# Last products with V moved ahead of router work at the end of attention, and three low pieces of the first weights moved behind the first index lists

## The reference

```python
# attention, 8 heads of 64: keys within 16 positions, and 24 blocks of 32 keys (max of k, mean of v)
a = softmax(concat(mask(scale * q @ k.T), scale * q @ k_sum.T + log(32)))
x = a @ concat(v, v_sum)
# first mixture: 8 experts, the best two of noisy logits
logits = x @ w_gate + log1p(exp(x @ w_noise)) * noise
for e in range(8):                      # top2_w: softmax over the two
    out[mask] += top2_w * (relu(x[mask] @ w1[e]) @ w2[e])
# second mixture: one expert per token, and only where x @ w_skip > 0; out = x + gate * expert(x)
```

## Time and profile before

| | |
|---|---|
| median of 3 runs | 667.83 us (665.47 to 668.64) |
| the profiled execution's own time | 665.87 us |
| its span in the profile | 663.4 us |
| PE busy | 620.8 us, 94% of the span |
| DVE busy | 367.9 us, 55% |
| ACT busy | 293.9 us, 44% |
| POOL busy | 237.9 us, 36% |

### The profile page before, as it was taken

One profiled execution on the slowest core, in us unless ns is written; L12 is line 12 of the kernel. 1 busy time (PEld: TensorE's weight loads), 2 busy tenths in 40 slices (PEclk: granted clock), 3 DMA queues, 4 the chain that ended last, 5 costly groups with the idle time before them and its releaser, 6 DMA issues.

```text
span 663.4 us, 13555 instructions
## 1 busy us (share of the span) xinstructions
PE 620.8 (94%) x4054; PEld 551.5 (83%) x4054; DVE 367.9 (55%) x714; ACT 293.9 (44%) x536; POOL 237.9 (36%) x223
## 2 busy tenths in 40 slices
PE   6888848999999999999999999998699999999994
PEld 6567735999999999999999999985478888888883
DVE  5759985644535554364644536423564687656641
ACT  2657732433424443253433434433255475646621
POOL 2558303105527063370725527033112223231230
PEclk9999967999999999999999999998699999999998
DMA  9999881442926448283672926885296679568220
GB/s 305 326 285 305 301 295 53 155 152 55 269 66 180 140 93 264 54 213 94 150 207 54 273 65 157 236 251 113 72 330 208 208 220 357 160 187 266 40 50 13
DMA packets 57633, 119.79 MB, mean 181 GB/s; under 512 B 13588, under 2 KB 13972, under 8 KB 57568
## 3 DMA queue, kind: packets, MB, share of 16 engines
q1 hardware_dynamic: 39424, 94.59, 43.4%
q0 software_dynamic: 14304, 23.93, 17.2%
q10 hardware_dynamic: 3840, 0.49, 0.5%
HBM read 103.51 MB, written 23.50 MB: 191 GB/s over the span
## 4 chain that ended last, share of the span: by engine, by line
PE 84%; DMA 5%; DVE 4%; issue 2%; SPq 2%; POOLq 0%; ACT 0%; POOL 0%; DVEq 0%; ACTq 0%
PE bank L964 22%; PE bank L856 22%; PE bank L850 22%; PE bank L839 2%; DMA q_ring<-in_q 2%; PE bank L819 2%; PE bank L745 2%; PE bank L980 2%; PE bank L724 1%; DMA xg<-x_moe,ix_take 1%; PE bank L768 1%; PE bank L758 1%; PE bank L713 1%; PE bank L936 1%; DVE col_val L1778 1%
## 5 line engine op out<-in xcount | busy, mean ns | idle before, releaser
L1615 DVE TENSOR_TENSOR w_lo<-stage,w_hi x120 | 141.7, 1222 | 22.9 <-ACT w_hi L1097 22.1
L1097 ACT CAST w_hi<-stage x120 | 119.7, 1050 | 9.0 <-PE bank L964 8.9
L856 PE MATMUL bank<-unit_hi,w_hi 128*128 128x416 f32 x256 | 92.6, 362 | 0.0
L1873 DVE SCALAR_TENSOR_TENSOR unit_lo<-bank,unit_hi 128x416 fp32r<-128x416 f32 x64 | 37.9, 592 | 96.8 <-ACT unit_hi L1211 96.8
L850 PE MATMUL bank<-tok_hi,w_hi 128*128 128x416 f32 x256 | 90.5, 354 | 0.6 <-DVE tok_lo L1825 0.6
L1211 ACT ACTIVATE unit_hi<-bank 128x416 fp32r<-128x416 f32 x64 | 33.2, 519 | 129.9 <-PE bank L850 129.9
L856 PE MATMUL bank<-unit_lo,w_hi 128*128 128x416 f32 x256 | 90.2, 352 | 0.0
L850 PE MATMUL bank<-tok_hi,w_lo 128*128 128x416 f32 x256 | 89.7, 350 | 0.0
L856 PE MATMUL bank<-unit_hi,w_lo 128*128 128x416 f32 x256 | 89.7, 350 | 0.0
L1429 POOL DMA_INDIRECT x_more<-more_out,ix_put x32 | 51.6, 1614 | 42.2 <-DVE more_out L1844 26.3
L1441 POOL DMA_INDIRECT x_moe<-rows_out,ix_put x32 | 55.2, 1726 | 9.8 <-issue 9.8
(11 more groups left out here) (162 smaller groups left out, 1072.5 us busy)
## 6 DMA issues: line engine op xcount, KB each, us to landing
stage<-in_moe_w SPq DMA_DIRECT2D x128, 512.0 KB, 5.6
v_win<-in_v SPq DMA_DIRECT2D x24, 198.0 KB, 8.9
v_raw<-in_v SPq DMA_DIRECT2D x6, 528.0 KB, 13.4
x_moe<-rows_out SPq DMA_DIRECT2D x12, 260.0 KB, 3.6
kt<-in_k SPq DMA_DIRECT2D x8, 384.0 KB, 9.0
q_ring<-in_q SPq DMA_DIRECT2D x6, 512.0 KB, 9.6
x_att<-x_sb POOLq DMA_DIRECT2D x12, 256.0 KB, 5.8
x_part<-x_moe SPq DMA_DIRECT2D x4, 768.0 KB, 8.8
```

The costliest lines, as they stand in the source:

```text
L856: last = eng.matmul(ps_out[chunk][:, 0:W], w[:, WC // 2 + f, chunk * P:(chunk + 1) * P], h[:, f % UNITS, :], start=(f == 0 and i == 0), st ...
L1097: eng.copy(piece(w_hi[n % SETS], j), stage[:, j, :]).then_inc(s_hi, 1)
L1615: eng.tensor_tensor(piece(w_lo[n % SETS], j), stage[:, j, :], piece(w_hi[n % SETS], j).bitcast(F32), ALU.subtract)\
L1873: eng.scalar_tensor_tensor(unit_lo[:, f % UNITS, :], ps_unit[f % 2][:, 0:W], 0.0, unit_hi[:, f % UNITS, :].bitcast(F32), ALU.max, ALU.subt ...
```

## The change

On PE in step 26, `times_v(23)` stands first, then `router_logits(9)`, then the turn of tile 10. As ACT's wait for `x_sb` of tile 11 then no longer covers tile 9's logits, `TAIL` is 3: tiles 9 to 11 are in the second part on ACT and DVE, and in the second PSUM bank. On DVE the low pieces 5, 6 and 7 of the first weights are no longer made in steps 23, 24 and 25. Pieces 5 and 6 come behind the register load ahead of the first `rest_of_x`, piece 7 behind the fourth.

```diff
-        TAIL = 2
+        TAIL = 3
...
+                last_v = s - PV_LAG == STEPS - 1
+                if last_v:
+                    times_v(STEPS - 1)
                 if (t := tile_at(s, GATE_LAG)) is not None and t < NT - 2:
...
                     router_logits(t)
-                if s - PV_LAG == STEPS - 1:
+                if last_v:
                     do_job(("x", NT - 2))
-                if 0 <= s - PV_LAG < STEPS:
+                elif 0 <= s - PV_LAG < STEPS:
                     times_v(s - PV_LAG)
...
-            SPLIT_AT = (13, 15, 17, 19, 21, 23, 24, 25)
+            SPLIT_AT = (13, 15, 17, 19, 21)
+            SPLIT_LATE, SPLIT_LAST = (5, 6), (7,)
...
                 eng.reg_load(counts, todo_i[0:1, 0:E])
+                for piece_no in SPLIT_LATE:
+                    split_first(piece_no)
                 for t in range(PARTS):
                     rest_of_x(0, t, ps_first[t])
+                for piece_no in SPLIT_LAST:
+                    split_first(piece_no)
```

## The result

The changed kernel takes 670.07 us in the median of 20 runs (665.08 to 674.78), the kernel before 666.87 (663.47 to 669.9, 20 runs). The ratio is 1.0058, with a 95% interval of 1.0037 to 1.0078: a loss of 2.5 to 5.2 us. The ratio and its interval are worked out from all runs of both kernels and need not be the quotient of the medians. The forecast of 668.5 had the sign and less than half of the size (+1.6 us on the mean that it stood on).

The account below looks back on a forecast made before the run. PE was taken to bound most of the kernel, and a relay of PE, ACT, DVE and gathers the touched stretch. Tail +0.6 and gather +1.0 made +1.6 us on a mean of 666.95: 668.5, range 665.6 to 671.4.

Parts of the forecast that it names:

- What bounds the stretch: End of attention to first round: a relay of PE, ACT and DVE, then the gathers; any shift moves all the rest.
- The tail, +0.6: End of attention on DVE: the three-tile tail waits for the last logits, `route` at 90.85 against 90.26, +0.6 us.
- ACT's copy ahead of the exponential: ACT at tile 10: the first exponential starts only when the copy ends, at 85.32, leaving 0.57 of 1.48 us.
- The splits that go and come cost nothing by themselves: DVE's low pieces: removal gains nothing by itself, the two new splits hide before the first `rest_of_x`, piece 7 costs nothing.
- The gather, +1.0: First mixture's third gather: two released 512 KB loads travel beside its rows, +1.0 us between bounds of 0 and 2.5.
- rival 3: First mixture's third gather: both pieces go whole ahead of it, 0.6 + 2.5 = +3.1 us, 670.1; chance 0.09.
- Rival 4: POOL's third and fourth gather instructions held by DVE's splits, at most one split each, +3.9 us, 670.9; chance 0.07.

Follow-up runs that it names:

- the kernel with one load: Changed kernel with SyncE holding the second set's piece 6 load, and so piece 7's, until the fourth gather landed; 667.5 against 665.25, ratio 1.0037.
- the kernel with the filled waits: Changed kernel with more products that only keep TensorE busy between the first turned parts (5, 7, 6, 3); 668.91 against 665.25, ratio 1.0053.
- the splits alone: Kernel before with only the three low pieces moved behind the index lists, old order and TAIL = 2; 668.21 against 664.75, ratio 1.0045.
- the loads alone: Kernel before, early splits, loads of pieces 5 and 6 held to the first gather's landing, piece 7's to the fourth's; 670.92 against 664.75, ratio 1.01.
- the splits and no traffic: Changed kernel with SyncE holding the second set's loads 5, 6 and 7 until the fourth first gather landed; 667.2 against 664.75, ratio 1.002.

## Why the prediction was right or wrong

- **What bounds the stretch**: right. PE, then ACT, then DVE, then the gathers; the head start of `times_v(23)` ended at ACT's copy of tile 10, and the tail of three tiles made DVE wait. Two of the forecast's signs were missed. Counted from the same mark, ACT's first exponential came at 85.06, where 85.2 to 85.4 was given, and `top_d` at 90.22, where 90.6 to 91.0 was.
- **The tail, +0.6**: right in its mechanism, too large by 0.6 in this profile. The last logits began 5.54 us behind `times_v(22)`, against 5.35 before: 0.19 late, where I had 0.35, as two `times_v` in a row take 1.09 us and not 1.24. And they took 1.06 us, at the high clock, with the exponential 1.10 behind their start; I had put in 1.5 because the clock fell within them before. Here it fell just behind them (at about 90). In the kernel with one load it fell as they began (86.3): they took 1.86 us there, and a was 9.10. In the kernel with the filled waits the clock was low for the products with V and again from 88.0, and a was 10.43. So over the five profiles with this order and the late splits the term is 0 in three, +0.7 in one and +2.1 in one. That 0.6 is near their mean is no merit of the forecast, which had one cause of one size.
- **ACT's copy ahead of the exponential**: the exponential started 0.48 us behind the copy's start, not behind its end at 0.59.
- **The splits that go and come cost nothing by themselves**: right. The pair ended at 110.84, 1.24 us ahead of the first `rest_of_x`, 1.18 us each; without the traffic they cost nothing in m. One reading in the forecast was wrong without harm: two splits of 1.80 us from 107.6 end at 111.2, and so wouldn't have been hidden by 111.0.
- **The gather, +1.0**: the collision was where it was forecast, but the term was mis-sized: it measured 2.2 and 2.7 us at the round's start in two profiles of the changed kernel, 2.6 with the filled waits, 3.2 with the splits alone, 4.5 with the loads alone, and 1.4 for one piece. A piece fills the engines for about 1.25 us. One piece costs about one such time, and two cost 2.2 us or more: the mechanism of rival 3, at 0.09, was what happened. Its sign, over 5.5 us to landing, is met by the fourth gather (5.63) and not by the third (5.0). I had set a share against the rows of the second mixture, which tell of landing times in traffic, and not of who goes first. What the Trainium skill says of arbitration ("DMA: Bandwidth & Descriptors", queues, rings and completion order), that an engine drains a whole packet of descriptors from one queue before it turns to the next, is in agreement with the 1.4 and 2.2 us and with the view of DMA, where in one stretch of 1 us 166 of the profile's packets (2 KB rows) were the load's and 9 the gathers'.
- **What the delay does to the clock**: not forecast at all. It cost +1.2 and +0.8 us in the changed kernel's two profiles, +1.0 with the loads alone and +2.0 with the splits alone. I weighed the clock for the logits and not for the round's start, where PE stands waiting for what I had just made late.
- **Rival 4**, POOL held by DVE: it did not happen, 942/1027/1120 ns against 937/1024/1117 before, and m of 71.0 with the splits and no traffic. The rule of the Trainium skill that stood beside it ("SBUF — State Buffer", SBUF: two separate sides) doesn't bite between these splits and these gathers.
- **The size of the whole**: 0.6 + 1.0 became 0 + 2.2 + 1.2. The time lies in the range because the range was wide, taken from the scatter of single runs, and that it falls on rival 3's 670.1 is luck in part: that sum had 0.6 for a tail that gave 0, and nothing for the clock.

## What to carry to other kernels

An instruction that seems free because its engine is idle may still be what holds a load back: before it is moved, ask for each semaphore that it raises which transfer that lets go, and what else is in flight then. Here a load that nobody waited for cost its full length and more (1.4 us for one of 1.25) when it went ahead of a gather that everybody waited for. And the delay of the first input of a long run of products cost twice where it was long enough, by itself and by the clock that fell while TensorE waited.

## What the runs showed of the hardware that was not expected

- Two loads of 512 KB, each 1.25 us of the engines at 418 GB/s, delayed a 32-row gather by 2.6 us in the changed kernel (3.06 to 5.67 us from its issue to its use) and the round by 4.5 us where they were issued as the first gather landed. The last is nearly twice what their bytes need: one or two of the sixteen DMA engines finished their part of a gather 1.5 us and more behind the others.
- The granted clock falls at other places from profile to profile, though the code of the stretch is the same: in the 12 profiles, it fell in or ahead of the last logits in some and behind them in others. With the end of attention coded alike, a was 8.32 in three profiles, 9.10 in one and 10.43 in one.
- Whole times of one kernel scatter by 6 to 10 us, mostly from two stretches: from the start to the end of attention (`times_v(22)` between 80.7 and 86.6) and between the mixtures (83.0 to 87.8). The rounds between them repeat to 0.2 us.
